# Token mix in turned form: U products in column tiles, and h added onto turned x1 in PSUM

## The reference

```
def _moe_ref(x, mu_k, mu_r, w_k, w_v, w_r):            # channel mix
    xk = mu_k * x + (1.0 - mu_k) * x_prev
    xr = mu_r * x + (1.0 - mu_r) * x_prev
    v = np.maximum(xk @ w_k, 0.0) ** 2 @ w_v
    return sigmoid(xr @ w_r) * v                        # called x1 in the kernel

def _moe2_ref(x, U, V, w_ch1, w_ch2):                   # U (768, 32), V (32, 768)
    h = x.transpose(0, 2, 1) @ U @ V
    u = x + h.transpose(0, 2, 1)
    return u + np.maximum(u @ w_ch1, 0.0) @ w_ch2
```

## Time and profile before

| | us |
|---|---|
| median of 3 runs | 758.4 (757.46 to 760.63) |
| the profiled execution, its own time | 757.66 |
| its span in the trace | 755.9 |
| TensorE busy | 718.0 (95% of the span) |
| VectorE busy | 428.5 (57%) |
| ScalarE busy | 252.8 (33%) |
| GpSimd busy | 60.8 (8%) |

### The profile page before, as it was taken

One profiled execution on the slowest core, in us unless ns is written; L12 is line 12 of the kernel. 1 busy time (PEld: TensorE's weight loads), 2 busy tenths in 40 slices (PEclk: granted clock), 3 DMA queues, 4 the chain that ended last, 5 costly groups with the idle time before them and its releaser, 6 DMA issues.

```text
span 755.9 us, 22449 instructions
## 1 busy us (share of the span) xinstructions
PE 718.0 (95%) x10120; PEld 678.3 (90%) x10120; DVE 428.5 (57%) x751; ACT 252.8 (33%) x498; POOL 60.8 (8%) x123
## 2 busy tenths in 40 slices
PE   4777989999999999999999999999999999989998
PEld 4677979889999999979999999979999999969998
DVE  4788869772696338662496427754387525341312
ACT  1344545233424153233333234232442324321211
POOL 3401102000010001100021001100011000000000
PEclk9999989999999999999999999999999999999999
DMA  8655320003300051000500024000610000000000
GB/s 225 189 168 204 95 84 2 2 2 96 107 3 2 2 153 48 3 2 17 180 7 3 1 79 124 2 3 2 167 34 3 2 9 33 1 0 1 30 3 32
DMA packets 17647, 39.97 MB, mean 53 GB/s; under 512 B 2800, under 2 KB 8560, under 8 KB 17552
## 3 DMA queue, kind: packets, MB, share of 16 engines
q1 hardware_dynamic: 17456, 38.48, 17.1%
q10 hardware_dynamic: 96, 0.07, 0.0%
HBM read 32.64 MB, written 4.72 MB: 49 GB/s over the span
## 4 chain that ended last, share of the span: by engine, by line
PE 88%; DVE 5%; issue 2%; ACT 2%; DMA 1%; SPq 1%; POOL 0%; DVEq 0%; ACTq 0%
PE acc L615 13%; PE acc L616 12%; PE acc L617 12%; PE hps L615 12%; PE hps L616 11%; PE hps L617 11%; PE aps L438 5%; PE hps L703 2%; PE aps L570 2%; PE aps L589 2%; PE aps L449 1%; PE aps L547 1%; DVE QK L1065 1%; DMA QK<-in_q 1%; PE aps L525 1%
## 5 line engine op out<-in xcount | busy, mean ns | idle before, releaser
L1256 DVE SCALAR_TENSOR_TENSOR hid_l<-hps,hid_h 128x384 fp32r<-128x384 f32 x96 | 53.5, 557 | 195.1 <-ACT hid_h L951 195.0
L951 ACT ACTIVATE hid_h<-hps 128x384 fp32r<-128x384 f32 x96 | 47.2, 492 | 203.9 <-PE hps L617 195.7
L615 PE MATMUL hps<-in_h,w_h 128*128 128x384 f32 x288 | 99.0, 344 | 0.7 <-DVE in_l L1236 0.6
L616 PE MATMUL hps<-in_l,w_h 128*128 128x384 f32 x288 | 96.8, 336 | 0.0
L617 PE MATMUL hps<-in_h,w_l 128*128 128x384 f32 x288 | 96.8, 336 | 0.0
L616 PE MATMUL acc<-w_l,hid_h 128*128 128x384 f32 x288 | 96.6, 336 | 0.0
L615 PE MATMUL acc<-w_h,hid_h 128*128 128x384 f32 x288 | 96.6, 335 | 0.0
L617 PE MATMUL acc<-w_h,hid_l 128*128 128x384 f32 x288 | 96.3, 335 | 0.0
L1065 DVE TENSOR_TENSOR QK<-QK,T 112x768 f32<-112x768 f32 x80 | 77.1, 973 | 12.9 <-PE aps L438 11.6
L919 ACT ACTIVATE tmp<-hps 128x384 f32<-128x384 f32 x64 | 31.5, 493 | 148.9 <-PE hps L617 148.0
L1374 POOL TENSOR_TENSOR T<-T 112x384 f32<-112x384 f32 (+4 forms) x80 | 42.3, 532 | 473.9 <-DVE QK L1074 310.7
(11 more groups left out here) (123 smaller groups left out, 1251.2 us busy)
## 6 DMA issues: line engine op xcount, KB each, us to landing
QK<-in_k SPq DMA_DIRECT2D x16, 336.0 KB, 4.1
QK<-in_q SPq DMA_DIRECT2D x16, 336.0 KB, 4.7
T<-in_alpha SPq DMA_DIRECT2D x16, 336.0 KB, 7.2
vt<-in_v SPq DMA_DIRECT2D x16, 288.0 KB, 7.6
raw<-in_w_ch SPq DMA_DIRECT2D x6, 768.0 KB, 6.6
out<-x SPq DMA_DIRECT2D x24, 192.0 KB, 2.0
QK<-in_q_odd SPq DMA_DIRECT2D x16, 168.0 KB, 6.1
raw_k<-in_w_k SPq DMA_DIRECT2D x3, 512.0 KB, 4.9
```

The lines of the kernel that those rows point to most:

```text
L615: pe.matmul(o, a[0], b[0], start=first, stop=False)
L616: pe.matmul(o, a[0], b[1], start=False, stop=False)
L951: nc.scalar.activation(hid[0][:, f % 2, :], hps[f % 2][:, 0:HT], ACT.Relu).then_inc(s_rel2, 1)
L1256: nc.vector.scalar_tensor_tensor(out=hid[1][:, f % 2, :], in0=hps[f % 2][:, 0:HT], scalar=0.0, in1=hid[0][:, f % 2, :].bitcast(F32), op0=A ...
```

## The change

- **U products in column tiles.** For each chunk `mix_g` issues three products of 128 columns in place of one of 384. Feature block j goes to the partitions 32j to 32j + 31 of `hps[0]`. ScalarE casts g by three copies of 32x128, VectorE forms the low part by three, and the second copy stays whole.
- **Turned form.** u isn't formed in `x1` any more. TensorE turns x1 itself (`turn_x1`, transposes that leave the bank open for accumulation; half 0 now into the three `acc` banks) and adds h in turned form onto it, one product for each feature block: `g_stack`'s 128 columns stationary, `v_stack`'s 384 columns moving (`add_turned_h`). VectorE's six additions go.
- **h in the output.** Since `x1` lacks h, `add_h` puts it into `acc` ahead of each half's first sum of w2: three products with V's chunk, six a batch.
- **Memory.** `g_stack` gets memory of its own and shares it with `u_sb`, so U is loaded again for each later batch, in the queue behind the stores of the batch ahead; TensorE waits on `s_U` for it.
- **Order.** On TensorE step 8 (the sixth level) moves from behind the last sum of v to ahead of it, the chunks 0 to 2 of `mix_g` from ahead of it to behind it (in the last batch they stay ahead). VectorE keeps its order through the lists `BESIDE1_DVE` and `BESIDE_T_DVE`. On ScalarE the last step of the channel mix and the first of the token mix adjoin, so its order stays too.

```diff
-        u_sb = sb("u_sb", [P, NC, R])
+        with ExitStack() as first:
+            u_sb = early(first, "u_sb", [P, NC, R])
+        g_stack = sb("g_stack", [3 * R, DM], F32R)
...
-        g_stack = hid[0][0:3 * R, 0, 0:DM]
...
-            return (hps[0], hps[1], acc[2])[j] if half == 0 else (hps[0], aps[0], hps[1])[j]
+            return acc[j] if half == 0 else (hps[0], aps[0], hps[1])[j]
...
                 store((n - 2) // 2, n % 2)
+                if n % 2 == 1:
+                    sp.dma_start(u_sb[:], U).then_inc(s_U, 16)
...
+            def turn_x1(half, j):
+
+                for t in range(HC):
+                    pe.matmul(u_bank(half, j)[:, t * P:(t + 1) * P], x1[:, half * HC + t, j * P:(j + 1) * P], ident[:],
+                              start=t == 0, stop=False, is_transpose=True)
+
+            def add_turned_h(half, j):
+
+                pe.matmul(u_bank(half, j)[:, 0:HT], g_stack[:, j * P:(j + 1) * P], v_stack[:, half * HT:(half + 1) * HT],
+                          start=False, stop=True).then_inc(s_ut, 1)
...
-                    mm = pe.matmul(hps[0][0:R, 0:DM], u_sb[:, c, :], x1[:, c, :], start=(c == 0), stop=(c == NC - 1))
+                    for j in range(KT):
+                        mm = pe.matmul(hps[0][j * R:(j + 1) * R, 0:P], u_sb[:, c, :], x1[:, c, j * P:(j + 1) * P],
+                                       start=(c == 0), stop=(c == NC - 1))
...
-            def first_g(b):
-
+            def first_g(b, ahead):
+
+                if not ahead:
+                    yield
+                pe.wait_ge(s_U, 16 * (b + 1))
...
                 mix_g(b, range(HC, NC)).then_inc(s_g, 1)
+                for j in range(KT):
+                    turn_x1(0, j)
                 step(plan[1])
-                pe.wait_ge(s_gh, 2 * b + 2)
-                pe.wait_ge(s_gl, b + 1)
-
-                for c in range(HC):
-                    mix_h(c)
+                pe.wait_ge(s_gh, 4 * (b + 1))
+                pe.wait_ge(s_gl, KT * (b + 1))
+                for j in range(KT):
+                    add_turned_h(0, j)
                 step(plan[2])
-                pe.wait_ge(s_u, NC * b + HC)
-                turn_u(b, 0, 0, lambda: None)
-                turn_u(b, 0, 1, lambda: pe.wait_ge(s_rel, F1 * (2 * b + 2)))
-                turn_u(b, 0, 2, lambda: None)
-                for c in range(HC, NC - 1):
-                    mix_h(c)
+
+            def add_h(half):
+
+                for t in range(HC):
+                    c = half * HC + t
+                    pe.matmul(acc[t][:, 0:DM], v_stack[:, c * P:(c + 1) * P], g_stack[:], start=True, stop=False)
...
-                    if f == 0 and half == 0:
-                        mix_h(NC - 1)
                     if f > 0:
                         if f == 1:
                             acc_free()
+                            add_h(half)
...
-                nc.scalar.copy(g_stack[0:R, :], hps[0][0:R, 0:DM]).then_inc(s_gh, 1)
-                act.wait_ge(s_gh, 2 * b + 1)
+                for j in range(KT):
+                    nc.scalar.copy(g_stack[0:R, j * P:(j + 1) * P], hps[0][j * R:(j + 1) * R, 0:P]).then_inc(s_gh, 1)
+                act.wait_ge(s_gh, 4 * b + KT)
                 nc.scalar.copy(g_stack[2 * R:3 * R, :], g_stack[0:R, :].bitcast(F32)).then_inc(s_gh, 1)
...
-BESIDE1 = [1, 1, 1, 1, 1, 1, 0, 1, 0, 0]
-BESIDE_T = [1, 1, 1]
+BESIDE1 = [1, 1, 1, 1, 1, 1, 0, 1, 0, 1]
+BESIDE_T = [0, 1, 1]
+BESIDE1_DVE = [1, 1, 1, 1, 1, 1, 0, 1, 0, 0]
+BESIDE_T_DVE = [1, 1, 1]
```

More of the change, by code:

```diff
@@ L625, in hidden, with add @@
                 return mm
-            def add(w, f, n, done=None):
+            def add(w, f, n, done=None, ahead=False):
                 for t in range(HC):
@@ L633, in add, with turn_u @@
                     mm = three(acc[t][:, 0:DM], [x[:, f % 2, t * P:(t + 1) * P] for x in hid],
-                               [x[:, f, :] for x in w], f == 0, f == n - 1)
+                               [x[:, f, :] for x in w], f == 0 and not ahead, f == n - 1)
                 return mm
-            def turn_u(b, half, j, bank_free):
+            def turn_x1(half, j):
[5 more added lines that the diff above has]
+                          start=False, stop=True).then_inc(s_ut, 1)
+            def turn_u(half, j, bank_free):
                 bank_free()
[L639 to L642, removed]
+                turn_x1(half, j)
+                add_turned_h(half, j)
             def turn_half_u(b, free0, free2):
-                turn_u(b, 1, 0, free0)
-                turn_u(b, 1, 1, lambda: None if b == NB - 1 else kept(pe, 2 * b + 3, ML, 1))
-                turn_u(b, 1, 2, free2)
+                turn_u(1, 0, free0)
+                turn_u(1, 1, lambda: None if b == NB - 1 else kept(pe, 2 * b + 3, ML, 1))
+                turn_u(1, 2, free2)
                 yield
@@ L754, in mlp @@
                             low_ready(pe, W2_LOW[f // 2])
-                        add(w2, f - 1, F2).then_inc(s_out2, 1)
+                        add(w2, f - 1, F2, ahead=True).then_inc(s_out2, 1)
                 turns = iter(turns)
@@ L775, in _ @@
             run(steps)
-            pe.wait_ge(s_U, 16)
             for b in range(NB - 1):
@@ L1009, in _ @@
                 token_mix(b, step, BESIDE_T)
-                mlp(b, 0, step, BESIDE2, lambda: act.wait_ge(s_h, NC * (b + 1)), lambda: mix(b + 1, 0, 0))
+                mlp(b, 0, step, BESIDE2, lambda: act.wait_ge(s_out, F1 * (2 * b + 2)), lambda: mix(b + 1, 0, 0))
                 run(steps)
@@ L1240, in token_mix @@
                 step(plan[0])
[L1241 to L1249, removed]
+                for j in range(KT):
+                    cols = slice(j * P, (j + 1) * P)
+                    dve.wait_ge(s_gh, 4 * b + j + 1)
+                    nc.vector.tensor_tensor(g_stack[R:2 * R, cols], hps[0][j * R:(j + 1) * R, 0:P],
+                                            g_stack[0:R, cols].bitcast(F32), ALU.subtract).then_inc(s_gl, 1)
+                step(plan[1] + plan[2])
+                low_u(b, 0)
             def mlp(b, half, step, plan, next_mix=lambda: None, before_last=lambda: None, late=lambda f: None):
@@ L1322, in _ @@
             b = NB - 1
-            channel_mix(b, 1, alone, BESIDE1, lambda: gate(b, 1))
-            token_mix(b, alone, BESIDE_T)
+            channel_mix(b, 1, alone, BESIDE1_DVE, lambda: gate(b, 1))
+            token_mix(b, alone, BESIDE_T_DVE)
             mlp(b, 0, alone, BESIDE2, before_last=lambda: low_u(b, 1))
```

21 lines of the change are left out of this document (7 added, 14 removed).

## The result

| | before | changed |
|---|---|---|
| median, us | 757.93 (756.28 to 760.63, 4 runs) | 747.83 (746.76 to 748.43, 4 runs) |
| ratio | | 0.9862, 95% interval 0.9830 to 0.9893 |
| span of the traced execution | 755.9 | 746.7 |

The changed kernel is 10.1 us faster. Measured once more beside other runs of the kernel before, it took 747.92 against 757.97, ratio 0.9867 (0.9848 to 0.9885). The forecast was 748.8, with a range of 745.5 to 753.5.

What follows compares the result with a forecast made beforehand. TensorE's sequence, 88% of the chain that ended last, was taken as the bound. Three middle batches at 2.2 us (6.6) plus 2.6 in the last gave 9.2 saved; forecast 748.8 us, range 745.5 to 753.5.

Steps and rivals of the forecast that it cites:

- U products as column tiles: Each 384-column U product as three 128-column tiles running beside each other: 0.25 us a chunk, where one had streamed 0.65.
- Pairs only: Rival: matmuls start strictly in line, only neighbours overlap, 0.327 us a chunk, +1.8 us, 750.6; chance 0.14.
- tiles in line: Rival: U product tiles run one after the other with loads hidden, 0.65 us a chunk, +9.6, 758.4; chance 0.06.
- The rule that speaks against it: Skill's rule that weight loads overlap matmuls only in different row groups; U's column tiles share rows, so would go in line.
- slower rival: Column tiles of U products in line with every load laid bare: 1.31 us a chunk, +25, 774; chance 0.05.
- The path of a middle batch: TensorE's new order around the token mix: path 11.05 us to 7.45, net gain 2.2 after additions elsewhere, three times.
- A to H: Start of v's last sum's last matmul to the MLP's first hidden row: 6.2 us forecast, 4.5 in the last batch.
- turned k: TensorE turning k, in the new order between the nine turned blocks and the products with V: 1.30 us.
- the stop comes back as g's chain: Rival: small copies of g cost nearly what whole ones do, TensorE stops; +2 to +4 us, 752; chance 0.10.
- The sixth level: Moved ahead of v's last sum in middle batches: 1.27 us with lead and tail, hiding VectorE's last low part of v.
- Products paid elsewhere: Per batch: h added into both halves' sums 1.05 us, half 1's turned banks 0.52, one V product less -0.17; sum 1.4.
- The last batch: No attention beside it, first U group stays ahead of v's last sum: gain 2.8 + 1.2 - 1.4 = 2.6 us.

Runs made afterwards that it cites:

- one tile: Changed kernel with the same 18 U products of 128 columns all in partitions 0 to 31, g copied once: 758.34 us against 757.97, ratio 0.9989.
- order alone: Kernel before with only the sixth level moved ahead of v's last sum and all middle-batch U products behind it: 759.13 us against 757.80, ratio 1.0021.
- tiles alone: Kernel before with only the U products as three column tiles, with three copies and three low parts of g: 753.21 us against 757.80, ratio 0.9943.

## Why the prediction was right, point by point

**U products as column tiles.** Right. The 18 products took 1.44 us with lead and tail (1.51 as the view's row has them), a shade below "within 1.5 to 1.8". The chunk was mis-sized: 0.25 taken, 0.218 found. One record is 0.109 us and three tiles' records start within 13 ns of one another, so three run at once fully. I had scaled by the 2.6 and 3.1 of four tiles of the attention's short products; for these longer streams nothing was lost. Tail included, the group was forecast 0.16 us too long. "Pairs only" and "tiles in line" are out by the 1.44 us; "one tile" shows what in line would have cost, 4.04.

**The rule that speaks against it.** 36 loads of 32 columns, all on the same rows, recorded at 0.11 us each, fit into 1.44 us beside the matmuls. The rule of the Trainium skill that I had quoted, in "TensorE: Matmul & The Clock Gate", section "Part 3: Packing small matmuls", that loads overlap only where the row group differs, does not hold here, and the slower rival that it stood beside went with it.

**The path of a middle batch.** Right in its parts. Small copies: 0.82 for three on ScalarE and 0.92 on VectorE, where 0.87 for each was worked out between the 3-column and the 384-column row. VectorE's part of g ready at A+3.62 (3.65), ScalarE's at A+3.20 (3.4). A stop of 0.36 ahead of the chunk states from start to start (0.3; by the same measure 0.63 before), and none ahead of hidden. A to H 6.02 (6.2).

**The largest miss** of a middle batch is turned k: taken at 1.30 from the earlier trace rows, it lasts 1.08. The starts of single records tell why. Before and in "order alone" its second record starts 0.15 us behind its first, in the changed kernel 0.10: 0.05 was a lead behind the U products, which now stands in the blocks of x1. And the products with V start 0.19 behind its last record, where the changed kernel has 0.03. In all three batches of both kernels that start lies 0.146 to 0.147 us behind the end of VectorE's low part of g (155.13 in the earlier trace rows), just as the chunk states start 0.144 behind the end of ScalarE's copies of turned k. So 0.16 of the 1.30 was a short stop on g, which the view doesn't mark, and the prediction read it as work.

The cover of g's chain was thinner than forecast, too. VectorE is done with its part 0.22 us before the products with V start (0.45 forecast), and 0.15 of that passes between its end and a start anyway: 0.07 are left. With three low parts at the price of a whole one, 0.55 in place of 0.28, it would have been 0.8 us later (an estimate). So the rival "the stop comes back as g's chain" was near, and the small copies' low price kept it away.

**The sixth level.** Its move hid v's last low part as planned: no stop ahead of the last sum (147.69, 150.17 above). X to A is 2.75 us, where 1.27 for the level and 1.58 for nine products make 2.85.

**Products paid elsewhere.** 1.4 forecast, 1.43 to 1.52 found.

**The last batch.** 2.6 forecast; 4.11 - 1.44 = 2.67 found, A to H 4.48 for 4.5, with stops of 0.34 and 0.81.

**The reload of U.** No wait on it. Its issue follows the stores, SyncE queue in order of time, for the earlier trace rows:

```profile
283.12 1.38 SPq L358 DMA_DIRECT2D out<-x  x3
284.54 0.46 SPq L428 DMA_DIRECT2D u_sb<-in_U  x1
```

It landed within 3.8 us (median of four) and was asked for at 323.

**The sum.** 9.2 forecast, 9.8 from the stages and 10.1 from the medians. In a middle batch the products (0.16) and turned k (0.22) were taken too long, the blocks of x1 (1.04 us for 0.96) and the products with V with the stop behind them (0.97 for 0.82) too short. That and 0.1 at the sixth level make the net gain 2.4 for 2.2. The stages thus account for 0.6 of the 1.0 us by which the median lies below the forecast; the rest is below what medians can tell. That the total came out so close owes something to these misses of either sign.

| | tiles: no | tiles: yes |
|---|---|---|
| old order, before's form | 757.9 | 753.2 |
| new order, before's form | 759.1 | not run |
| old order, turned form | not run | 751.2 |
| new order, turned form | 758.1 | 747.8 |

What the prediction did not say is how the 10 us divide. The parts don't add up: tiles 4.6, the rest nothing, together 10. With the tiles in place the turned form brings 2.0 (753.2 to 751.2), and the order on top of it 3.4 (751.2 to 747.8); what the order would bring to the tiles without the turned form was not run. The tiles shorten what covered ScalarE's chain, and the order takes its longest piece out of that chain.

## What to carry to other kernels

A product with a stationary side of 32 columns can be cut along its moving side into three tiles of columns that run at once; the price is a result in three blocks, which the next step must take in that form. Before making a covered stretch shorter, ask whose chain it covered: here all that the second group of products saved (1.27 us a batch), and 0.3 more, came back as stops on ScalarE, an engine a third busy, until its four copies were moved ahead of the chain. And where the end of an opening scatters by 2 us, compare stages from start to start: 0.5 us is plain there, and can't be seen in medians.

## What the runs showed of the hardware

**Matmuls of different column tiles overtake.** With three products on one tile in a row, 36 records took 2.02 us, where strict order would need some 3.4 (an estimate from the 0.109 us between records on one tile) and alternating tiles took 1.44. Alternate the tiles in the stream.

**The clock in the last batch.** In the traced run of "tiles alone" TensorE stopped 1.47 and 1.23 us with 0.8 us of products between, and from within the second stop on it was granted half its clock, the 1.2 GHz level, for 6.8 us; four windows around the place, with each engine's busy time and the granted clock (PEclk):

```profile
core 0: us, PE busy (x) PEld busy (x) DVE busy (x) ACT busy (x) POOL busy (x), PEclk, DMA share, GB/s
665.00:669.00 4.00, 2.13 (x23) 0.97 (x22) 2.43 (x7) 1.28 (x4) 0.00 (x0) 1.00 0.00 0
669.00:673.00 4.00, 3.09 (x13) 3.10 (x14) 2.33 (x5) 1.44 (x3) 0.00 (x0) 0.54 0.00 0
673.00:677.00 4.00, 4.00 (x17) 4.00 (x16) 2.13 (x5) 0.49 (x1) 0.00 (x0) 0.61 0.00 0
677.00:681.00 4.00, 4.00 (x25) 4.00 (x24) 0.67 (x2) 0.65 (x2) 0.00 (x0) 1.00 0.00 0
```

A matmul of 384 columns lasts 0.52 us there for 0.34, and its last H to end is 81.03 for 79.45. This run took 755.3. The kernel's other three took 752.8 to 753.5 and have no trace, but most likely it didn't happen in them: their mean clock of 0.991 allows 13.5 us at half clock, which the opening's last two such stretches (6.8 us each in the trace) use up. The kernel before, with stops of 1.23 and 1.23 us in the same place but longer U products ahead of them, kept the full clock in its trace. In this trace the last batch lost 1.6 us behind H, more than the 1.1 that its shorter U products had saved ahead of it; that the stops caused it is likely and not shown. In the changed kernel the stops there are 0.34 and 0.81 and the clock stayed full in both traces.
